# Attention with hash buckets and two feed-forward layers: order of the first pair's rounding, of the q and k loads, and of the one-hot steps

## What is computed

```python
q_bits = (np.einsum('bhsd,dk->bhsk', q, proj) > 0).astype(np.int64)
q_bucket = np.sum(q_bits * powers, axis=-1)           # the same for k
mask = q_bucket[:, :, :, None] == k_bucket[:, :, None, :]
scores = np.where(mask, scale * q @ k.T, -1e9)
attn = exp(scores - max); attn = attn / (sum + 1e-9)
x = (attn @ v), heads side by side: 1536 x 512
x = g1(x @ w_in) @ w_out        # g1 a ratio of polynomials, width 2048
out = g2(x @ w_in2) @ w_out2    # g2(h) = h - tanh(h)
```

## Time and profile before

| | |
|---|---|
| median of 3 runs | 751.3 us (750.47 to 751.36) |
| the profiled execution | 751.21 us, of which the span of the profile is 749.4 us |
| PE busy | 734.7 us, 98% of the span |
| PEld, DVE, ACT, POOL busy | 624.8, 605.0, 484.1, 272.5 us |
| mean granted clock of TensorE | 0.998 |
| data moved by DMA | 60.21 MB, nearly all by SP's queue |

### The profile page before, as it was taken

One profiled execution on the slowest core, in us unless ns is written; L12 is line 12 of the kernel. 1 busy time (PEld: TensorE's weight loads), 2 busy tenths in 40 slices (PEclk: granted clock), 3 DMA queues, 4 the chain that ended last, 5 costly groups with the idle time before them and its releaser, 6 DMA issues.

```text
span 749.4 us, 11868 instructions
## 1 busy us (share of the span) xinstructions
PE 734.7 (98%) x3715; PEld 624.8 (83%) x3715; DVE 605.0 (81%) x931; ACT 484.1 (65%) x938; POOL 272.5 (36%) x249
## 2 busy tenths in 40 slices
PE   7998999999999999999999999999999999999998
PEld 4997998998998888788888888888888788888886
DVE  5987998888997999999988888975685698875622
ACT  7887888988897878788766867755553233322321
POOL 6685566566569000000000000000058499992000
PEclk9999999999999999999999999999999999999999
DMA  6758668768745500000000032320000110000101
GB/s 200 176 154 200 186 165 196 192 165 197 165 124 157 188 1 0 1 1 1 1 1 14 30 113 84 111 88 14 1 1 28 43 43 28 15 15 0 57 1 56
DMA packets 43612, 60.21 MB, mean 80 GB/s; under 512 B 7088, under 2 KB 25776, under 8 KB 43568
## 3 DMA queue, kind: packets, MB, share of 16 engines
q1 hardware_dynamic: 43424, 59.26, 29.3%
q10 hardware_dynamic: 144, 0.39, 0.1%
HBM read 31.66 MB, written 3.19 MB: 47 GB/s over the span
## 4 chain that ended last, share of the span: by engine, by line
PE 72%; DVE 10%; SPq 6%; POOL 5%; issue 4%; DMA 3%; ACT 1%; POOLq 0%; ACTq 0%; DVEq 0%
PE acc L867 31%; PE h_ps L833 18%; PE h_ps L957 9%; PE slot L266 5%; PE turn_ps L378 4%; PE pv_ps L342 2%; PE pv_ps L344 2%; DMA kA<-k_hot 2%; SPq L1388 2%; DVE sqr L1155 1%; DVE pol L1176 1%; SPq L1390 1%; DVE pol L1162 1%; SPq L1386 1%; DVE pol L1187 1%
## 5 line engine op out<-in xcount | busy, mean ns | idle before, releaser
L780 POOL TENSOR_TENSOR wout_raw<-win_hi 128x256 f32<-128x256 f32 x8 | 8.9, 1137 | 319.6 <-DVE win_lo L1208 309.2
L608 DVE TENSOR_TENSOR pt_lo<-turn_ps,pt_hi 128x384 fp32r<-128x384 f32 x192 | 97.8, 552 | 16.9 <-ACT pt_hi L522 16.6
L522 ACT ACTIVATE pt_hi<-turn_ps 128x384 fp32r<-128x384 f32 x192 | 85.2, 495 | 26.6 <-PE turn_ps L378 26.1
L833 PE MATMUL h_ps<-x_hi,win_lo 128*128 128x512 f32 x256 | 99.9, 390 | 0.0
L833 PE MATMUL h_ps<-x_lo,win_hi 128*128 128x512 f32 x256 | 99.6, 389 | 0.0
L833 PE MATMUL h_ps<-x_hi,win_hi 128*128 128x512 f32 x256 | 99.6, 389 | 0.0
L566 DVE TENSOR_REDUCE row_min<-slot 128x1 f32<-128x768 f32 x96 | 90.9, 948 | 5.8 <-PE slot L266 5.3
L996 ACT ACTIVATE g_hi<-pol 128x512 fp32r<-128x512 f32 x80 | 50.9, 637 | 66.5 <-PE acc L867 34.1
L454 ACT ACTIVATE E<-slot,row_min 128x768 f32<-128x768 f32 x96 | 87.4, 911 | 2.0 <-issue 1.7
L1200 DVE TENSOR_TENSOR g_lo<-pol,g_hi 128x512 fp32r<-128x512 f32 x80 | 65.9, 824 | 21.7 <-ACT g_hi L996 21.4
L378 PE MATMUL turn_ps<-ident,E 128*128 128x128 f32 x576 | 80.6, 274 | 0.4 <-DVE pt_lo L608 0.3
(11 more groups left out here) (192 smaller groups left out, 1811.4 us busy)
## 6 DMA issues: line engine op xcount, KB each, us to landing
win_raw<-in_moe_w_in SPq DMA_DIRECT2D x32, 256.0 KB, 3.3
wout_raw<-in_moe_w_out SPq DMA_DIRECT2D x32, 256.0 KB, 2.8
v_nat<-in_v SPq DMA_DIRECT2D x8, 384.0 KB, 4.1
q_t<-in_q SPq DMA_DIRECT2D x7, 384.0 KB, 3.1
k_t<-in_k SPq DMA_DIRECT2D x7, 384.0 KB, 3.7
qA<-q_hi SPq DMA_DIRECT2D x14, 192.0 KB, 3.7
qB<-q_hi SPq DMA_DIRECT2D x14, 192.0 KB, 4.0
qB<-q_lo SPq DMA_DIRECT2D x14, 192.0 KB, 4.1
```

Source lines behind the costliest of these rows:

```text
L522: eng.activation(pt_hi[:, c % 2, k0:k0 + T // 2, i * P:(i + 1) * P], turn_ps[h][:, 0:HALF].rearrange("r (k n) -> r k n", n=P), ACT.Copy).t ...
L608: eng.tensor_tensor(pt_lo[dst], turn_ps[h][:, 0:HALF].rearrange("r (k n) -> r k n", n=P), pt_hi[dst].bitcast(F32), ALU.subtract).then_inc( ...
L833: mm = eng.matmul(h_ps[t % 4][:, :], w[:, ws], columns(x, kt, c), start=kt + n == 0, stop=kt == KT - 1 and n == 2)
```

## The change

In the prologue ACT rounds k (kA) directly behind the first rounding of q, instead of behind all three operations on q, and DVE makes the remainder of k (kB) behind its copy, waiting for kA; POOL keeps only the remainder of q. In the pairs, SP issues the two loads of pair p + 2 behind `load_v(p + 1)`, instead of ahead of `copy_split(p + 1, 0)`. The projection moves to step 0 and the one-hot parts to steps 1 to 4 (in pair 0 to steps 1 and 2 to 5). ACT scales q in step 9 instead of 8, ACT prepares the row sums of the first head in step 5 instead of 4, and DVE takes their reciprocals in step 6 instead of 5.

```diff
--- before.py
+++ after.py
@@ -77,7 +77,7 @@
              for name in ["ident", "consts", "coefs", "ready", "coef", "proj", "q", "k", "v", "out", "ops0", "ops1",
                           "scale_out0", "scale_out1", "scale_in0", "scale_in1", "shift0", "shift1", "pool_here", "sync_here"]
              + ["t_first_q", "t_first_k", "t_q", "t_dots", "t_bits", "t_hot", "t_hot_q", "t_hot_k",
-                "t_hi_q", "t_hi_k", "t_hi_kb", "t_lo", "t_op1", "t_zeros"]
+                "t_hi_q", "t_hi_k", "t_hi_kb", "t_lo", "t_lo_k", "t_op1", "t_zeros"]
              + [f"w_in{j}" for j in range(J)] + [f"w_out{j}" for j in range(J)]}
     mlp_sems = {name: top.enter_context(nc.semaphore("m_" + name)) for name in
                 ["h", "g2", "acc", "square", "ln", "r0", "tanh", "g_hi", "w_in_hi", "w_out_hi",
@@ -198,8 +198,8 @@
 
 
 
-        DOT_STEP = 1
-        HOT_STEPS = {2: (0, 0), 3: (1, 0), 4: (0, 1), 5: (1, 1)}
+        DOT_STEP = 0
+        HOT_STEPS = {1: (0, 0), 2: (1, 0), 3: (0, 1), 4: (1, 1)}
         G = T // 2
         GROUPS = TILES // G
 
@@ -317,7 +317,8 @@
             eng.wait_ge(loads["t_hi_q"], 2)
             eng.wait_ge(loads["t_hi_k"], 1)
             eng.wait_ge(loads["t_hi_kb"], 1)
-            eng.wait_ge(loads["t_lo"], 2)
+            eng.wait_ge(loads["t_lo"], 1)
+            eng.wait_ge(loads["t_lo_k"], 1)
             eng.wait_ge(loads["t_hot_q"], 2)
             eng.wait_ge(loads["t_hot_k"], 2)
             pe_scores(eng, 0, 0)
@@ -349,9 +350,7 @@
         def pe_att(eng, p, first=False, prepare=True, turn=True, last=False):
             for n in range(TILES - G * last):
                 pe_tile(eng, p, n)
-                if first and n == 2:
-                    pe_dots(eng, 1)
-                if prepare and not first and n == DOT_STEP:
+                if prepare and n - first == DOT_STEP:
                     pe_dots(eng, p + 1)
                 if prepare and n - first in HOT_STEPS:
                     pe_hot(eng, p + 1, *HOT_STEPS[n - first])
@@ -408,13 +407,13 @@
             eng.wait_ge(loads["t_first_q"], 16)
             eng.activation(opA[0][0][0:D, :], first_qk[0][0:D, :], ACT.Copy,
                            scale=-1.0 / float(D) ** 0.5).then_inc(loads["t_hi_q"], 1)
+            eng.wait_ge(loads["t_first_k"], 16)
+            eng.activation(opA[0][1][0:D, :], first_qk[1][0:D, :], ACT.Copy
+                           ).then_inc(loads["t_hi_k"], 1)
             eng.activation(first_q[:, :], first_qk[0][:, :], ACT.Copy,
                            scale=-1.0 / float(D) ** 0.5).then_inc(loads["t_q"], 1)
             eng.activation(opB[0][0][D:2 * D, :], first_qk[0][0:D, :], ACT.Copy,
                            scale=-1.0 / float(D) ** 0.5).then_inc(loads["t_hi_q"], 1)
-            eng.wait_ge(loads["t_first_k"], 16)
-            eng.activation(opA[0][1][0:D, :], first_qk[1][0:D, :], ACT.Copy
-                           ).then_inc(loads["t_hi_k"], 1)
             eng.wait_ge(loads["consts"], 32)
             for e in range(2):
                 o = D - e * D
@@ -524,11 +523,11 @@
                                    ACT.Copy).then_inc(sems["pt_hi"], 1)
                 if first and n == 0:
                     act_scale(eng, 1)
-                if turn and n == 8:
+                if turn and n == 9:
                     act_scale(eng, p + 2)
                 if n + AHEAD - 1 < TILES or not last:
                     act_exp(eng, p, n + AHEAD - 1)
-                if n in (4, 9 if last else 11):
+                if n in (5, 9 if last else 11):
                     act_sum(eng, p, n // T)
                 if prepare and HOT_STEPS.get(n - first, (0, 0))[0] == 1:
                     act_hot_k(eng, p + 1, HOT_STEPS[n - first][1])
@@ -547,6 +546,9 @@
             hs = [slice(0, HALF), slice(HALF, S)]
             eng.wait_ge(loads["t_first_k"], 16)
             eng.tensor_copy(opB[0][1][0:D, :], first_qk[1][0:D, :]).then_inc(loads["t_hi_kb"], 1)
+            eng.wait_ge(loads["t_hi_k"], 1)
+            eng.tensor_tensor(opB[0][1][D:2 * D, :], first_qk[1][0:D, :],
+                              opA[0][1][0:D, :].bitcast(F32), ALU.subtract).then_inc(loads["t_lo_k"], 1)
             eng.wait_ge(loads["t_dots"], 1)
             eng.tensor_scalar(bits[:, :], slot[0][:, 0, 0:HALF], 0.0, None, ALU.is_gt
                               ).then_inc(loads["t_bits"], 1)
@@ -609,15 +611,13 @@
                                       turn_ps[h][:, 0:HALF].rearrange("r (k n) -> r k n", n=P),
                                       pt_hi[dst].bitcast(F32), ALU.subtract
                                       ).then_inc(sems["pt_lo"], 1)
-                if n in (5, 9 if last else 11):
-                    dve_scale(eng, p, n // T)
+                if n in (6, 9 if last else 11):
+                    dve_scale(eng, p, int(n > T))
                 if last and n == TILES - 3:
                     dve_step(eng, 0)
                 if last and n == TILES - 2:
                     dve_sum(eng, GROUPS - 2)
-                if first and n == 2:
-                    dve_bits(eng, 1)
-                if prepare and not first and n == DOT_STEP:
+                if prepare and n - first == DOT_STEP:
                     dve_bits(eng, p + 1)
                 if prepare and HOT_STEPS.get(n - first, (1, 0))[0] == 0:
                     dve_hot_q(eng, p + 1, HOT_STEPS[n - first][1])
@@ -645,13 +645,11 @@
         def pool_first(eng):
             source = [first_q, first_qk[1]]
             eng.wait_ge(loads["t_q"], 1)
-            for x in range(2):
-                lo_at = slice(0, D) if x == 0 else slice(D, 2 * D)
-                eng.wait_ge(loads[("t_hi_q", "t_hi_k")[x]], 1)
-                eng.tensor_tensor(opB[0][x][lo_at, :], source[x][0:D, :],
-                                  opA[0][x][0:D, :].bitcast(F32), ALU.subtract
-                                  ).then_inc(loads["t_lo"], 1)
-                eng.wait_ge(loads["t_lo"], x + 1)
+            eng.wait_ge(loads["t_hi_q"], 1)
+            eng.tensor_tensor(opB[0][0][0:D, :], first_q[0:D, :], opA[0][0][0:D, :].bitcast(F32),
+                              ALU.subtract).then_inc(loads["t_lo"], 1)
+            eng.wait_ge(loads["t_lo"], 1)
+            eng.wait_ge(loads["t_first_k"], 16)
 
             mine = slice(D, 2 * D)
             for x in range(2):
@@ -1456,15 +1454,15 @@
                                       ).then_inc(loads["out"], 16)
 
                 def sync_att(p, turn=True):
-                    if turn:
-                        load_qk(p + 2, 0)
-                        load_qk(p + 2, 1)
                     copy_split(p + 1, 0)
                     if not is_zero(p):
                         shift(p - 1, 1)
                     scale_out(p, 0)
                     copy_hot(p + 1, 0)
                     load_v(p + 1)
+                    if turn:
+                        load_qk(p + 2, 0)
+                        load_qk(p + 2, 1)
                     copy_split(p + 1, 1)
                     copy_hot(p + 1, 1)
                     scale_in(p, 0)
```

## The result

| | before | after |
|---|---|---|
| median | 751.36 us (5 runs) | 771.59 us (5 runs, 767.94 to 776.58) |
| ratio, 95% interval | | 1.0272 (1.0216 to 1.0328) |
| profiled execution / span | 751.21 / 749.4 us | 771.59 / 769.8 us |
| PE busy | 734.7 us | 741.7 us |
| mean granted clock | 0.998 | 0.988 |

The forecast was 754.0 us, with 757.0 as its upper end. The direction was right, and PE does wait for ACT, which waits for q, as the forecast has it; the size was far off. Of the 20.4 us by which the span grew, 7.0 are PE being busy longer for the same matmuls, 13.4 are PE idle.

What follows compares the result with a forecast made beforehand. The preparation circle, 27.82 us a turn, paced pairs 1 to 5. Growing to 28.47, with q late, it put pair 6's first tile 2.9 us later: 751.2 + 2.8 = 754.0 us; own range 752.3 to 756, whole range 748.3 to 757.0.

Steps and rivals of the forecast that it cites:

- POOL's circle: POOL's split, SP's copies and v's load, second head's landing, POOL again: 27.82 us a turn, pacing pairs 1 to 5.
- its second part: From the end of k_lo to the second head's landing, on SP and full DMA engines: 20.2 us.
- Against that stand the gaps, of which I let the load fill 0.45. So the circle grows by 0.65 us: q's load behind v costs 1.09 us at 362 GB/s, less 0.45 in DMA gaps; bounds 1.09 and -0.3 us.
- q at 8.9: On SP's queue, q's load was to be issued 8.9 us after the end of k_lo, behind v.
- In the loop it is ready before SP arrives: The later first-head reciprocal, awaited by SP's scale_out, was priced at 0, with 0.5 us either way.
- the next T is not before K + 18.3: The next pair's first tile comes at least 18.3 us after the end of k_lo, against 17.5 before.
- I take v's 4.1 and land it at K + 13.0: q's load takes 4.1 us from issue, as v's did, landing 13.0 us after the end of k_lo.
- slower still, on ACT: Rival: q takes 5.1 us in the queue, no gap is filled, ACT waits; 6.1 us later, 757.3 us; chance 0.12.
- First head's copies sooner: With k's load gone from the queue's front, k_hot is issued 1.3 us sooner.
- two issues taking it back: The two loads behind v put 1.3 us of issuing ahead of the second head's copies.
- steps at nothing: Projection and one-hots one step earlier, with the same instructions, were priced at nothing.
- prologue at 0.1 us: Before the pairs, DVE's new subtraction and POOL's lost one: 0.1 us booked, between -0.8 and +0.4.

Runs made afterwards that it cites:

- e9: The kernel before plus one 384 KB load that nobody reads, behind the load of v in pairs 0 to 5: 758.73 us, ratio 1.0092.
- e11: The kernel before with k's load behind v and an extra 384 KB load nobody reads there too, q's own load early: 760.43 us, ratio 1.0117.
- e2: The kernel before with only SP's loads of q and k moved behind the load of v: 769.18 us, ratio 1.0225.
- e4: The change with the row sums back in step 4 and the reciprocal in step 5, loads still late: 763.43 us, ratio 1.0153.
- e3: The change with ACT's scaling of q in step 11 instead of 9, all else as changed: 766.98 us, ratio 1.0201.
- e1: The change with SP's loads of q and k put back ahead of the first head's copies: 751.75 us, ratio 0.9995.
- e7: The kernel before with k's load alone moved behind the load of v: 751.14 us, ratio 0.9994.
- e6: The kernel before with the change's prologue alone (ACT's order, DVE's subtraction for k): 750.98 us, ratio 0.9991.

## Why the prediction was wrong

**What bounds the kernel: right.** POOL's circle at 27.82 us was the limit, and every kernel that put bytes into its second part grew with it (e9, e11).

**"Against that stand the gaps, of which I let the load fill 0.45. So the circle grows by 0.65 us": too small.** e9 measures 1.5 us, e11 1.6, above even my upper bound of 1.09. 362 GB/s was read from 1.3 us in which the load stood first in a queue that was nearly empty (a share of 0.27 just before); in the full stretch 0.393 MB in 1.5 us are 262 GB/s, nearer the 236 of the whole stretch. Little of the gaps was filled: between the end of k_lo and the second head's landing the DMA share is 0.86 to 0.90 before and 0.92 to 0.93 in e11.

**"q at 8.9" and "In the loop it is ready before SP arrives": the step that failed.** I tied q's issue to K, the end of k_lo, and set the wait for the first head's reciprocal ahead of it to nothing. Before, that is so: SP issues scale_out 0.35 us after the shift in each of pairs 1 to 5. In the change this takes 0.7 to 3.2 us, and in e2, whose reciprocal has not moved, 0.5 to 2.2. I had not asked what SP waits for once PE is delayed. Where SP stands there, q's issue hangs on the pair's own first tile (19.9 us after it) and not on K. So a second chain closed, which does not pass through POOL, and what PE lost came again in each pair. In pair 2 K is 80.92 + 1.84 = 82.76 and q goes out at 93.22, K + 10.5; in the five pairs it is K + 9.4 to K + 11.6, in e2 K + 9.3 to K + 12.0. My formula "the next T is not before K + 18.3" gives 101.1; the next pair's first tile came at 107.91. Of these 6.9 us q's issue has 1.6, its landing 3.0 and the way from the landing to the tile, which PE goes at the lower clock, 2.2. Over the five pairs T comes 19.6 us later than the formula: 7.7 by the issue, which is what SP stood at scale_out beyond those 0.35 us, 5.0 by the landing and 6.9 behind it. In pair 4, the one of the five in which the clock stayed at 1.00, the last part is 0.1. e4 gives 8 us back with the reciprocal alone, because it opens one step more between the reciprocal and the scaling.

**"I take v's 4.1 and land it at K + 13.0": under-sized.** q took 4.4 us in the median and 7.1 at the longest, v ahead of it only 3.3 and k behind it 6.1: here the later load paid. The Trainium skill, "DMA: Bandwidth & Descriptors", section "Anatomy of one DMA", has a fit for a DMA from GpSimd, with no term for what is queued ahead; by it 384 KB take 2.9 us, an estimate. The trace does not agree for q in the full stretch. The rival "slower still, on ACT" named the right wait and priced it at 6.1 us, because it too counted K and one wait, not a chain.

**Nothing in the sum for the clock.** Four of these six stalls of PE were followed by work at the lower clock. e3, whose longest stall in the pairs is 2.3 us, has PE busy 738.0 us at a clock of 0.998; e2 and the change have 742.7 and 741.7 at 0.987 and 0.988.

**First head's copies sooner, two issues taking it back; steps at nothing; prologue at 0.1 us.** e1, e7 and e6 bear these out to within 0.1% of the time. In e7 k_hot goes out 7.5 us after K, as forecast (7.4), yet PE waits 7.3 us for it in all against 5.0 before, so the relief is not collected there either. That the earlier one-hots cost nothing holds only while the copies are on time: in e3 DVE is held 5.9 us by them.

## What to carry to other kernels

Before a transfer is moved later in a hand-written queue, list what each wait ahead of it now hangs on: a load that hung only on the projection and on POOL's split came to hang on a reciprocal, which hung on the very engine that the load feeds. Count the steps between what releases such a transfer and what asks for it: at three steps ACT waited 14 to 17 us here, at five 1.5 us. An in-order engine that waits for it turns a late transfer into a closed chain, whose delay comes again in each turn. Price a transfer in a full stretch by that stretch's whole rate, not by its best microsecond.

## What the runs showed of the hardware

In the stall of 5.2 us the granted clock was still 1.00 from 97 to 100 us and stood at 0.51 from 100 to 107, with PE at work from 102.15. After some shorter stalls it was low as well, and only once PE was at work again: after the stall of 2.2 us that ended at 68.17 it was 1.00 until 69 and 0.50 from 70 to 72. After the stall of 1.5 us it stayed at 1.00, and so it did after one of 2.66 us, though not after one of 2.55 us: the length of the stall alone did not decide it here. And landings spread widely in a full queue: in its late place the same 384 KB of q took from 4.1 to 7.1 us. The changed kernel's runs lie 8.6 us apart, those of e9, where nobody waits for a late load, 2.2; that the spread of the landings is the cause is likely but not shown.
